# Fused attention and two feed-forward layers on one core: the first transfers issued in another order

## What is computed

```python
# attention: batch 4, heads 8, sequence 576, head width 64
scores = q @ k^T / 8
psi    = log1p(|i - j|) / log1p(max(i, 1))           # i, j: positions 0..575
bias   = relu(psi * w1 + b1) @ w2                    # 32 hidden units -> one 576x576 table per head
attn   = softmax(scores + bias)
x      = attn @ v                                    # -> 2304 tokens x 512
# first layer, 512 -> 768 -> 512
x = max(x @ w1, x @ w2, x @ w3) @ w_out, with relu on the maximum
# second layer, 512 -> 2048 -> 512
h = x @ w_in;  g = h where h >= 1, 0 where h <= -1, else (h + 1)^2 / 4;  out = g @ w_out
```

## Time and profile before

| | |
|---|---|
| median of three runs | 1095.83 us (1095.35 to 1095.99) |
| the profiled execution | 1096.08 us, its span 1094.1 us |
| PE busy over the span | 95% |
| bias stage | about 6 to 63 us |
| first steps of attention | about 62 to 104 us |
| PE busy from 700 to 1090 us | 389.53 of 390 us |

### The profile page before, as it was taken

How to read it: one execution, slowest core, us unless ns; L and a number is a source line. 1 busy time by engine, 2 the same in 40 slices (tenths; PEclk the granted TensorE clock), 3 DMA queues, 4 the chain that set the end, 5 groups by cost and what they waited for, 6 DMA issues and landing times.

```text
span 1094.1 us, 18925 instructions
## 1 busy us (share of the span) xinstructions
PE 1043.6 (95%) x6936; PEld 924.9 (85%) x6936; DVE 550.8 (50%) x1314; ACT 504.0 (46%) x1081; POOL 303.8 (28%) x536
## 2 busy tenths in 40 slices
PE   5859999999999999999999999999999999999998
PEld 3448777777777789999999999998999999989897
DVE  7838677776767622222223132774444454444543
ACT  6957666676667633121212132554343343443433
POOL 3028677776767554000000023660000000000000
PEclk9979999999999999999999999999999999999999
DMA  4771251342423033000000011320000000000000
GB/s 128 233 206 45 48 149 34 85 112 51 119 63 81 19 118 108 1 0 0 0 0 0 0 39 59 97 77 30 1 1 29 0 29 0 0 29 0 30 1 29
DMA packets 93156, 56.00 MB, mean 51 GB/s; under 512 B 61344, under 2 KB 78752, under 8 KB 93088
## 3 DMA queue, kind: packets, MB, share of 16 engines
q1 hardware_dynamic: 93088, 55.11, 17.6%
HBM read 39.46 MB, written 15.63 MB: 50 GB/s over the span
## 4 chain that ended last, share of the span: by engine, by line
PE 84%; DVE 9%; issue 2%; SPq 1%; ACT 1%; DMA 1%; POOL 1%; ACTq 0%
PE ps L1007 39%; PE ps L1067 18%; PE ps L1035 7%; PE ps L913 7%; PE ps L933 5%; PE ps L945 5%; DVE s_sb L746 3%; DVE xT L797 2%; DVE k_lo L764 2%; PE ps L898 2%; DMA bias_scratch<-p_t 1%; DVE pt_t L755 1%; PE ps L972 1%; PE ps L993 0%; ACT p_t L541 0%
## 5 line engine op out<-in xcount | busy, mean ns | idle before, releaser
L1007 PE MATMUL ps<-x_hi,w_all 128*128 128x384 f32 x1632 | 437.2, 336 | 0.3 <-issue 0.3
L1007 PEld LDWEIGHTS ps<-x_hi,w_all 128*128 128x128 f32 x1632 | 297.0, 188 | 5.3 <-issue 1.0
L1007 PE MATMUL ps<-x_lo,w_all 128*128 128x384 f32 x816 | 273.3, 335 | 0.0
L1067 PE MATMUL ps<-w_all,g_hi 128*128 128x512 f32 x576 | 179.8, 393 | 0.0
L746 DVE CUSTOM_DVE_ANT_0 s_sb<-ps,bias_h 128x576 f32<-128x576 f32 (+1 forms) x160 | 120.3, 753 | 87.2 <-PE ps L933 70.2
L1007 PEld LDWEIGHTS ps<-x_lo,w_all 128*128 128x128 f32 x816 | 153.2, 188 | 3.9
L502 POOL TENSOR_TENSOR w_all<-raw,w_all 128x256 fp32r<-128x256 f32 x104 | 80.3, 802 | 273.9 <-ACT w_all L622 269.7
L578 ACT ACTIVATE probs<-s_sb,row_min 128x576 f32<-128x576 f32 (+1 forms) x160 | 124.6, 779 | 34.4 <-DVE row_min L746 32.9
L469 POOL TENSOR_SCALAR probs<-probs,row_inv 128x512 f32<-128x512 f32 (+1 forms) x160 | 108.2, 689 | 87.3 <-DVE row_inv L726 87.3
L1067 PEld LDWEIGHTS ps<-w_all,g_hi 128*128 128x128 f32 x576 | 106.3, 188 | 19.2 <-issue 1.2
L945 PE MATMUL ps<-ident,probs 128*128 128x128 f32 (+1 forms) x640 | 93.3, 269 | 26.1 <-DVE k_lo L764 13.4
(11 more groups left out here) (87 smaller groups left out, 1384.6 us busy)
## 6 DMA issues: line engine op xcount, KB each, us to landing
bias_scratch<-p_t SPq DMA_DIRECT2D x36, 296.0 KB, 3.7
bias_h<-bias_scratch SPq DMA_DIRECT2D x32, 288.0 KB, 4.2
raw<-in_moe_w_out SPq DMA_DIRECT2D x22, 256.0 KB, 3.1
raw<-in_moe_w SPq DMA_DIRECT2D x18, 256.0 KB, 3.0
out<-o_sb SPq DMA_DIRECT2D x18, 256.0 KB, 2.1
q_in<-in_q SPq DMA_DIRECT2D x32, 128.0 KB, 2.3
k_in<-in_k SPq DMA_DIRECT2D x32, 128.0 KB, 2.4
v_in<-in_v SPq DMA_DIRECT2D x32, 128.0 KB, 2.3
```

Of the source, the lines that this page charges most:

```text
L1007: last = pe.matmul(ps[:, bank, 0:BLK], w[:, at:at + P], x[:, kt, :], start=(kt == 0 and n == 0), stop=(kt == KT - 1 and n == 2))
L1067: last = pe.matmul(ps[:, O_BANK + t, :], g[:, ft % 4, t * P:(t + 1) * P], w[:, wout_d(ft):wout_d(ft) + DM], start=(opens and i == 0), stop ...
```

## The change

Four things move. The counts of SP that open the four `bias_o` buffers stand first in SP's list. Of the four transfers of b1, the last two are issued by ACT, at the start of its list. The loads of q and k of pair 1 move from ahead of the stores to behind store 3, those of v to behind store 6, and those of pairs 2 and 3 from behind all bias loads to behind stores 22 and 23. And ACT's part of `step(-1)` stands one slab earlier.

```diff
+            for e in range(4):
+                sp.sem_inc(bias_free[e], 16)
             for r in range(G4):
                 lanes = slice(r * HID, (r + 1) * HID)
                 sp.dma_start(w1c[lanes, :], w1.rearrange("a k -> k a")).then_inc(small_in, 16)
+            for r in range(2):
+                lanes = slice(r * HID, (r + 1) * HID)
                 sp.dma_start(b1c[lanes, :], b1.rearrange("(k a) -> k a", a=1)).then_inc(small_in, 16)
...
             load_qk(0)
-            load_qk(1)
-            load_v(0)
-
-
-            for e in range(4):
-                sp.sem_inc(bias_free[e], 16)
...
             for s in range(NSUP):
                 store_bias(s)
+                if s == 3:
+                    load_qk(1)
+                if s == 6:
+                    load_v(0)
                 if s >= 4 and (s - 4) % 8 == 7:
                     first_bias((s - 4) // 8, s - 3)
+                if s in (NSUP - 14, NSUP - 13):
+                    load_qk(s - NSUP + 16)
...
-            load_qk(2)
-            load_qk(3)
             for i in range(PAIRS // 2):
...
         def _(act):
 
+            for r in range(2, G4):
+                lanes = slice(r * HID, (r + 1) * HID)
+                act.dma_start(b1c[lanes, :], b1.rearrange("(k a) -> k a", a=1)).then_inc(small_in, 16)
             act.wait_ge(a_rows, 1)
...
                 hidden_act(s)
                 bias_copy(s - 2)
-                if s == TURN + 2:
+                if s == TURN + 1:
                     step(-1)
```

## The result

The changed kernel took 1085.99 us (median of 4 runs, 1085.68 to 1088.05), the kernel before beside it 1095.59 us (4 runs, 1094.01 to 1095.99): ratio 0.9919, 95% interval 0.9902 to 0.9936. The forecast was 1085.6 us. Run again unaltered in a later comparison it took 1086.07 us (6 runs) against 1095.44, ratio 0.9927 (0.9912 to 0.9942). In that comparison two of the eleven executions of the kernel before were far longer (1476.4 and 2082.5 us); its median and the ratios are not moved by them.

The account below looks back on a forecast made before the run. Bounds taken: PE's 9.29 us wait for POOL at the seam, and waits at the start of the bias stage. Seam 9.6 plus start 0.65 gave 10.25 us off 1095.83, so 1085.6 us, range 1083.5 to 1088 (chance 0.57).

Parts of the forecast that it names:

- The term of the seam: Between bias stage and attention: an earlier split of pair 2 frees POOL, so PE's transposes start 9.6 us earlier.
- The term of the start: Bias stage: 4.05 us gained from earlier issues and fewer waits, less costs of 1.0 and 2.4 us, leaving +0.65 us.
- The upper end of the range: Seam: at most 11 us gained, if PE's clock does not fall and 3.06 us shrink by up to 1.5.
- ACT's lead of 1.2 us: Bias stage: ACT gains 5.25 us against DVE's 4.05, a lead that covers ACT's stalls behind late stores.
- term (b): Bias stage: loads of pair 1 and v hold SP 2.3 us each; ACT loses 0.5 to 0.7 us twice.
- (a): Bias stage: POOL's split of pair 2 runs beside DVE's slabs and slows them, costing 1.0 us.
- (c): Bias stage: loads of pairs 2 and 3 hold SP around one store; ACT loses 2.2 to 2.4 us.
- The sign named for (c): Store landings after slabs 22 and 23 over 5 us, an ACT wait of about 2 us at slab 28's copy.
- B: Bias stage: loads amid stores delay landings and starve the store ring; start gives -3, 1089.2 us; chance 0.19.
- D: Bias stage: SP becomes the bound, issues cost 9.3 us and bytes 6; slower, 1098.4 us; chance 0.03.
- A: Bias stage is also freed: start gives 3.5 us and seam 9.6, 1082.7 us; chance 0.18.
- C: Seam: another wait, such as late bias rows of head 1, takes the gain; start gives nothing, 1095.8 us; chance 0.03.

Follow-up runs that it names:

- s1_seam: The kernel before with only the loads of pairs 2 and 3 moved behind stores 22 and 23: 1088.33 us, ratio 0.9937.
- s2_start: The changed kernel with the loads of pairs 2 and 3 back behind the bias loads: 1092.88 us, ratio 0.9983.
- first profile: Profiled execution of the changed kernel in its first comparison, its longest run: 1088.05 us.
- second profile: Profiled execution of the changed kernel run again unaltered in a later comparison: 1086.35 us.
- c4_issue: The kernel before with ten added transfers of 128 bytes, five behind store 22 and five behind store 23: 1098.45 us, ratio 1.0031.
- s5_single: The changed kernel with the sixteen moved loads issued singly, behind stores 3 to 10, 13 to 16 and 21 to 24: 1082.94 us, ratio 0.9892.
- c3_turn: The changed kernel with ACT's part of `step(-1)` a slab later again: 1087.03 us, ratio 0.9926.
- c5_gap: The changed kernel with DVE waiting before slabs 3 and 11 for POOL's first instruction of splits 0 and 1: 1085.71 us, ratio 0.9923.

## Why the prediction was right

The total was met within 0.4 us. The term of the seam is right in mechanism and size. The term of the start came out near its sum partly by luck: two of its costs were divided wrongly, and the errors cancel.

**The seam, 9.6 us forecast, 9.0 to 9.35 measured.** The mechanism is shown from both sides: s1_seam has it alone, s2_start without it has the wait back. The third split lies at 49 us, PE's wait is gone, and the transposes come 7.6 us behind the last store's issue (63.32 us), where about 7 was forecast. The working let the bias blocks land no later than before; DVE's wait for the fourth block of pair 0 rose from 0.37 to 0.66 and 0.77 us, which is part of the missing 0.25 to 0.6. The upper end of the range, a clock that does not fall, did not come in the first profile:

```profile
46.00:62.60 16.60, 12.68 (x237) 7.93 (x229) 11.80 (x23) 13.11 (x20) 2.46 (x3) 0.90 0.85 238
...
70.00:79.00 9.00, 8.54 (x49) 8.09 (x50) 6.00 (x18) 6.51 (x18) 6.88 (x14) 0.70 0.71 201
```

The last three columns are granted clock, DMA share and GB/s. PE was busy 8.54 of 9 us there, at clock 0.70 on average, against none at 0.50 before.

**The start, +4.05 forecast before its costs.** It stood at 4.7 us at k_lo. Then about 1 us went where the prediction saw none: a stall of ACT of 1.4 us, that the kernel before also has (1.37 us, at the same shape), passes on to DVE as 1.20 to 1.46 us where it had been 0.40. The prediction let ACT's lead of 1.2 us (5.25 against 4.05) cover such stalls, and term (b). This lead never came about: ACT's first copy started at 9.49 us and not at about 8.7, since it waited for PE's first product,

```profile
9.49 0.76 ACT L546 ACTIVATE p_t<-ps,nconst 128x592 f32<-128x592 f32 x1 [1.27 <-PE ps L998]
```

so ACT was 13.38 - 9.49 = 3.9 us ahead of before, and not 5.25. The stalls of term (b), forecast at 0.5 to 0.7 us each, were 0.76 and 0.95 us in the first profile (slabs 8 and 11) and 0.43 and 0.11 in the second, and were not covered. At the slab of 449 elements 3.1 to 3.85 us of DVE's lead were left.

**(a) The split beside DVE, 1.0 us forecast; 1.06 measured in DVE's own time, about nothing in the stage's.** DVE's instructions by shape in the first profile, 44 to 60 us, against the earlier trace rows of before, which has 543 ns for this shape:

```profile
L802 DVE TENSOR_SCALAR xT<-log_t,row_sc,nb 128x513 f32<-128x513 f32 x3 | 2.5, 895 | 0.0
...
L802 DVE TENSOR_SCALAR xT<-log_t,row_sc,nb 128x497 f32<-128x497 f32 x3 | 1.4, 534 | 0.0
```

3 x (895 - 543) = 1.06 us. By the rule of the Trainium skill that was weighed beside it ("SBUF — State Buffer", section "Who interferes with whom") the whole split of 1.95 us would have been lost; DVE lost about half of that. But in the sum this term belongs at nothing, since DVE did not set the pace there. In the second profile:

```profile
50.29 0.76 ACT L546 ACTIVATE p_t<-ps,nconst 128x592 f32<-128x592 f32 x1 [1.87 <-DMA bias_scratch<-p_t]
...
53.02 0.75 ACT L546 ACTIVATE p_t<-ps,nconst 128x592 f32<-128x592 f32 x1 [1.28 <-DMA bias_scratch<-p_t]
53.67 0.80 ACT L537 ACTIVATE xT<-log_t,b1c,row_sc 128x513 f32<-128x513 f32 x1
```
```profile
54.57 1.21 PE L998 MATMUL ps<-xT,w2b 128*32 128x296 f32 x24 [1.53 <-DVE xT L802]
```

DVE's three slowed instructions are those of 513 elements, of slab 31. They were done before 52.48 us, where DVE's row of 18 instructions from 43.32 us ends, and that row includes slab 32. ACT's part of slab 31, behind its two stalls, is done only at 54.47 us, and PE's product of the slab starts 0.1 us later. So PE waited for ACT here, though the bracket names DVE, and the 1.06 us lay inside ACT's stalls.

**(c) The pair loads, 2.4 us forecast, about 3.4 measured.** Against the kernel before, ACT's copies are 3.85 us ahead at slab 26 (46.99 against 50.84 us), 0.46 at slab 28 and 0.47 at slab 35 in the second profile; 3.07, -0.35 and -0.63 in the first. So 3.4 us are lost at the copies of slabs 27 and 28. The forecast for (a) and (c) together was 3.4, from the lead at 449 elements to the end of the stage 3.50 us (second profile) and 3.8 (first) were lost: the sum is right because (c) was 1 us too small and (a) 1 us too large. c4_issue, in which no split runs beside DVE, agrees: its copies lose 3.2 us on the kernel before from slab 26 to 35. The mechanism of (c) is the one that the working gave, SP's issue time in a block. Its size was wrong because the eight loads were counted as one block with one stall; there were two, one behind each group:

```profile
51.00 0.75 ACT L546 ACTIVATE p_t<-ps,nconst 128x592 f32<-128x592 f32 x1 [1.80 <-DMA bias_scratch<-p_t]
53.83 0.75 ACT L546 ACTIVATE p_t<-ps,nconst 128x592 f32<-128x592 f32 x1 [1.38 <-PE ps L998]
```

The first is the copy of slab 27, the second of slab 28, in the first profile; the second ended with the landing of store 24 at 53.74 us. The sign named for (c), landings of over 5 us behind stores 22 and 23, did not show: between 43 and 56 us a store takes 3.2 to 4.9 us to land, median 3.8, against 3.1 to 4.0 in the same stretch before. The stores were issued late: 23 and 24 left SP 2.85 and 4.63 us after their copies had ended, against 0.03 us before.

**The rivals.** B (the ring starves by bytes, 1089.2) fell with c4_issue, where the stalls came without the bytes, and s5_single, where the bytes came without the stalls. Its working also had the bytes too high: it put all sixteen moved loads into this stretch, where eight stand. D's mechanism, SP's issues, is the real one, at a fraction of its price: about 3.4 us for the eight issues of pairs 2 and 3, and about 0.8 for the other eight, where it had 9.3 for the sixteen and 6 more for bytes. A (the stage freed as well, 1082.7) is false for this order and true for that of s5_single, which gave 1082.9, with the end of the stage 3.8 us and the seam 9.0 us better than before. C did not occur.

One thing is only argued. The runs of the changed kernel have a few 2 to 3 us above the rest (1088.05, 1089.41). In the first profile the clock is at the lower level behind the stall of the pair loads, after stretches in which PE did nothing:

```profile
54.00:55.00 1.00, 0.00 (x0) 0.00 (x0) 1.00 (x3) 1.00 (x2) 0.00 (x0) 0.98 1.02 320
55.00:58.00 3.00, 2.62 (x32) 1.57 (x36) 0.68 (x2) 3.00 (x6) 0.00 (x0) 0.50 0.98 292
58.00:59.00 1.00, 1.00 (x28) 0.60 (x23) 1.00 (x3) 1.00 (x3) 0.00 (x0) 0.81 0.86 294
```

DVE's wait for PE there is 2.32 us, against 1.23 in the second profile, where the granted clock is 1.00 from 46 to 62.6 us with stalls of the same size: some 1.1 us. That the longer runs without a profile have this cause is not shown. Another cause stands beside it: in the long executions that were profiled of two other orders (1095.14 us in s2_start, 1091.41 in c3_turn, 2.3 and 4.4 us above their medians) POOL's first instruction was held for over 13 us, and DVE waited 4.6 and 8.3 us for ACT's copy of k. Which of the two lengthens the other runs stays open.

## What to carry to other kernels

When an engine waits at a seam, look in which order the loads and the engine's own list stand, and ask what was ready long before; moving a load to where its buffer is free cost here little but its issues. Count those issues in the issuing queue against the slack of the transfers behind them, and spread them one at a time; a block of four cost here what the bytes did not. The largest wait in a table (here 4.5 us) may be worth nothing while a second wait, or the other engine of a pair, stands right behind it. And a term that is there in an engine's busy time (here DVE's 1.06 us) costs nothing while another engine of the pair is the later one: look for both parts of the slab before adding it to a sum.

## What the runs showed that was not expected

The first instruction of a split on POOL, 0.45 us when alone, took 1.99 us (split 0) and 4.18 us (split 1) in the first profile and, for split 0 in two others, 13.53 and 13.43 us beside DVE's hidden values. In the profile of s2_start, DVE's row and POOL's second instruction:

```profile
5.50 17.25 DVE L802 TENSOR_SCALAR xT<-log_t,row_sc,nb 128x576 f32<-128x576 f32 x39
```
```profile
23.03 0.72 POOL L459 TENSOR_SCALAR k_dup<-k_in 128x640 f32<-128x640 f32 x1
```

DVE ran 39 instructions without a gap until 22.75 us, and POOL's instruction from 9.53 us ended at 23.06, just behind. The 4.18 us of the first profile end at 24.16 us, behind DVE's stop at 5.51 + 18.33 = 23.84; in c5_gap, with a wait on DVE, that of split 0 took 0.48 us, and that of split 1 ended 0.31 us after DVE stopped. Where POOL is kept out, DVE loses nothing: these 39 instructions take 17.25 us, and 18.33 where the split came through at 9.66 to 13.50 us, 1.08 us more, the same price as in (a). So the two share in either of two ways, and what decides it the runs did not show. The Trainium skill, "SBUF — State Buffer", section "Who interferes with whom", says of VectorE in a two-port mode and GpSimd that whoever issues first gets the shared pair of ports for the whole instruction and the other fully blocks. No row tells which mode DVE's instructions are in. The trace agrees that POOL can be blocked fully, but here for some 30 instructions of DVE in a row and not one.

The second surprise is how little a transfer's size has to do with its issue: five of 128 bytes hold SP for 3.17 and 2.46 us, the four of pair 2, of 128 and 16 KB, 0.60 + 0.86 + 0.59 + 1.31 = 3.36 us in the first profile, those of pair 3 0.59 + 0.54 + 0.60 + 0.52 = 2.25. The Trainium skill, "Perfetto Trace Analysis", section "Optimizing DMA Performance", names the issuing engine's sequencer as one of the places where a kernel can be bound by DMA. This case agrees: SP issues without a gap of over 0.1 us from 43.4 to 53.1 us in the first profile, and that is where the stores fall behind.
